# Two expert layers behind induced attention: x pooled in runs of 16 points per partition, and layer two's up weights converted by ScalarE and VectorE

## What is computed

```python
B, N, m, C = 2, 11456, 32, 128; E, F = 8, 1024

def mab(q, kv):                      # attention, scale 1/sqrt(C)
    s = scale * (q @ kv.T); a = exp(s - s.max(-1)); a /= a.sum(-1) + 1e-9
    return a @ kv
h = mab(inducing, x)                 # 32 rows per batch: the pooling over all points
x = mab(x, h).reshape(B * N, C)      # every point

# layer one: expert by cosine with expert_emb, / tau
# layer two: logits = x @ w_gate + modality_bias[modality_id]
e = argmax(logits); gate = softmax(logits)[e]
out = gate * (relu(x @ w1[e]) @ w2[e])
```

## Time and profile before

| what | us |
|---|---|
| median of 3 runs | 1101.46 (1101.04 to 1102.66) |
| the profiled execution | 1104.6 |
| its span, in which all times of the trace lie | 1102.8 |
| mean granted TensorE clock, share of full speed | 0.954 |

### The profile page before, as it was taken

The page is one execution under the profiler, slowest core; times in us unless marked ns, Lnnn a source line. Parts: engine busy times, 40 slices in busy tenths (PEclk is TensorE's granted clock), DMA queues, the critical chain, the costliest instruction groups (busy, mean ns, idle before and its releaser), DMA issues.

```text
span 1102.8 us, 27898 instructions
## 1 busy us (share of the span) xinstructions
PE 987.3 (90%) x6367; PEld 498.8 (45%) x6367; DVE 760.5 (69%) x2224; ACT 666.7 (60%) x1614; POOL 248.8 (23%) x461
## 2 busy tenths in 40 slices
PE   5566473789999999999999999999999999999887
PEld 4445231345444444444444444444454444444433
DVE  3545575657778687777777787777777777877654
ACT  3434163456666666766666666666666666667553
POOL 2759911211111111111111111111111111111100
PEclk9868786789999999999999999999999999999999
DMA  9999372101111101010111111010101111010000
GB/s 194 301 282 297 124 244 67 31 21 28 38 33 28 42 23 47 23 47 24 40 30 37 34 26 44 23 47 23 44 26 38 32 30 41 23 47 23 16 23 21
DMA packets 75163, 70.71 MB, mean 64 GB/s; under 512 B 33370, under 2 KB 61570, under 8 KB 75118
## 3 DMA queue, kind: packets, MB, share of 16 engines
q1 hardware_dynamic: 75118, 70.14, 23.8%
HBM read 40.55 MB, written 23.55 MB: 58 GB/s over the span
## 4 chain that ended last, share of the span: by engine, by line
PE 81%; DMA 8%; POOL 4%; issue 2%; DVE 2%; ACT 1%; SPq 1%; ACTq 0%; DVEq 0%; POOLq 0%
PE y L1273 43%; PE up L1296 22%; PE up L1286 7%; DMA GW<-in_x 3%; DMA wraw<-in_moe_w 2%; PE y L1350 2%; POOL wraw L472 2%; PE TB L1312 1%; DMA x_turned<-GW 1%; POOL W1B L476 1%; PE TB L1336 1%; PE SM L1324 1%; PE up L1212 1%; PE SM L1344 1%; DMA ind<-in_inducing 1%
## 5 line engine op out<-in xcount | busy, mean ns | idle before, releaser
L856 DVE SCALAR_TENSOR_TENSOR hlo<-up,hhi 128x500 f16<-128x500 f32 x736 | 494.0, 672 | 171.5 <-ACT hhi L594 168.7
L594 ACT ACTIVATE hhi<-up 128x500 f16<-128x500 f32 x736 | 424.5, 583 | 170.6 <-PE up L1296 84.6
L1296 PE MATMUL up<-ytb,W1B 128*128 (+1 forms) x1104 | 276.4, 381 | 11.9 <-issue 11.3
L1273 PE MATMUL y<-hhi,W2A 128*128 128x500 f16 x736 | 218.5, 379 | 10.4 <-DVE hlo L856 5.5
L1273 PE MATMUL y<-hhi,GW 128*128 128x500 f16 x736 | 215.4, 374 | 0.4 <-DVE hlo L856 0.4
L1296 PEld LDWEIGHTS up<-ytb,W1B 128*128 x1104 | 108.7, 99 | 149.0 <-issue 40.3
L1286 PE MATMUL up<-E4T,GW 128*128 (+1 forms) x368 | 139.4, 382 | 0.0
L1273 PE MATMUL y<-hlo,W2A 128*128 128x500 f16 x368 | 138.7, 377 | 0.0
L1273 PE MATMUL y<-hlo,GW 128*128 128x500 f16 x368 | 137.5, 374 | 0.0
L1273 PEld LDWEIGHTS y<-hhi,W2A 128*128 x736 | 68.2, 98 | 92.9 <-issue 46.2
L514 POOL TENSOR_TENSOR st<-ss,root 125x4 f32<-125x4 f32 x46 | 46.9, 1019 | 236.4 <-ACT TB L620 236.4
(11 more groups left out here) (165 smaller groups left out, 1066.0 us busy)
## 6 DMA issues: line engine op xcount, KB each, us to landing
wraw<-in_moe_w SPq DMA_DIRECT2D x24, 512.0 KB, 4.7
xth<-x_turned SPq DMA_DIRECT2D x46, 250.0 KB, 2.6
out<-yout SPq DMA_DIRECT2D x46, 250.0 KB
x_turned<-GW SPq DMA_DIRECT2D x10, 1000.0 KB, 13.4
GW<-in_x SPq DMA_DIRECT2D x10, 960.0 KB
W1B<-in_moe_w SPq DMA_DIRECT2D x8, 512.0 KB, 11.9
x_turned<-GW SPq DMA_DIRECT2D x2, 750.0 KB, 9.7
GW<-in_x SPq DMA_DIRECT2D x2, 720.0 KB
```

Source lines behind the costliest of these rows:

```text
L594: nc.scalar.activation(hhi[:, (u % UP) * CT:(u % UP + 1) * CT], ups[u % UP][:, 0:CT], ACT.Relu).then_inc(s["hi_done"], 1)
L856: nc.vector.scalar_tensor_tensor(hlo[:, o:o + CT], ups[u % UP][:, 0:CT], 0.0, hhi[:, o:o + CT], ALU.max, ALU.subtract).then_inc(s["lo_done ...
L1273: ins = mm(y[:, 0:CT], W[:, bass.ds(woff + (fb * 2 * C + o), C)], h[:, k * CT:(k + 1) * CT], start=opens and fb == 0 and n == 0, stop=fb = ...
L1296: ins = mm(ups[k][:, 0:CT], W1B[:, bass.ds(woff + (wl * F + fb * P), P)], ytb[:, bass.ds(yoff + yl * CW, CT)], start=n == 0, stop=n == 2)
```

## The change

**Points.** A quad now is one run of 2000 points (1500 in the last of a batch): partition p holds 16 consecutive points (SPANS; 12 in the last), 8 KB, and chunk k of the quad is the points 4k to 4k + 3 of each partition. Quads start at STARTS. Within a batch only quad 3 (TWICE) overlaps its successor, by 44 points; `mix_points` leaves those out by its number of rows (`rows_kept`), and `keep_twice` sums their exponentials in two reductions, once for each batch. x is loaded as one DMA on 128 partitions (three more than are used), except for the last quad, where this would pass the end of x: it keeps 120 and 5 partitions. The turned quad is stored as one row of 8 KB per partition; modalities and results follow the same order of points (`points_of`). As the starts are numbers out of a table, SP's loop over the chunks is written out.

**Weights.** `w2a` and `w2b` are loaded with 4 KB per partition (eight consecutive rows of the matrix) instead of eight rows of 512 B. The hidden columns are thereby permuted, and the up weights follow: `high_low` reads `w1b` with a stride of eight elements, and the products' halves read PSUM with the same stride.

**Conversion.** `w1b` is halved by ACT (`high_up`) and DVE (`low_up`) in the pooling loop, expert e at the end of step q = e + 3. ACT first waits for POOL to be through with `w2a` of that expert, because W1B lies over its raw weights. `w1b` of expert e is loaded at q = e + 1, beside `w2a`. POOL halves only `w2a`; its one small power for the expert norms moves behind expert 1, and the steps that make and use the norms move from q = 0, 3, 4 and 5 to q = 2, 6, 7 and 8. `inducing` is loaded first, the small constants after the first four quads.

```diff
+    SPANS = [TJ * len(gs) for gs in CHUNKS]
+    TWICE = QB - 3
+    WITHIN = [sum(TQ * n for n in SPANS[0:k]) if k <= TWICE else NT - sum(TQ * n for n in SPANS[k:QB])
+              for k in range(QB)]
+    STARTS = [b * NT + r for b in range(NB) for r in WITHIN]
+    KEPT = WITHIN[TWICE + 1] - WITHIN[TWICE]
...
+        W1B_FROM = 3
...
+        def points_of(a, g, p0, p1):
+            q, k = quad_of(g)
+            rows = a[STARTS[q] + p0 * SPANS[q]:STARTS[q] + p1 * SPANS[q]]
+            return rows.rearrange("(p t) n -> p (t n)", t=SPANS[q])[:, k * TJ * a.shape[1]:(k + 1) * TJ * a.shape[1]]
+        def pieces(q):
+            whole = TQ // 8 * 8
+            return [(0, P)] if STARTS[q] + P * SPANS[q] <= NB * NT else [(0, whole), (whole, TQ)]
+        def rows_kept(q, k, j):
+            return -(-(KEPT - k * TJ - j) // SPANS[q]) if q % QB == TWICE else TQ
...
             if kind == "w1":
-                return dst[:, bass.ds(o, F)], dst[:, bass.ds(o + F, F)], a
+                return (*(dst[:, bass.ds(o + k * F, F)].rearrange("p (f c) -> p f c", c=P) for k in range(2)),
+                        a.rearrange("p (c f) -> p f c", f=NF))
...
             def load_points(q):
-                gs, slot, whole = CHUNKS[q], q % XR_N, TQ // 8 * 8
-                for p0, p1 in ((0, whole), (whole, TQ)):
-                    r0 = row0(sp, gs[0]) + p0 * TJ
-                    points = bass.AP(xf.tensor, r0 * C, [[TJ * C, p1 - p0], [STEP * C, len(gs)], [1, TJ * C]])
-                    sp.dma_start(xr[p0:p1, slot, 0:len(gs), :], points).then_inc(s[f"x_loaded{slot}"], 16)
+                slot, n = q % XR_N, SPANS[q]
+                for p0, p1 in pieces(q):
+                    sp.dma_start(xr[p0:p1, slot, 0:n * C],
+                                 xf[STARTS[q] + p0 * n:STARTS[q] + p1 * n, :].rearrange("(p t) c -> p (t c)", t=n)).then_inc(
+                        s[f"x_loaded{slot}"], 16)
             def load_w2a(e):
-                sp.dma_start(as_w2(w2raw[:, e, :]), w2a[e, :, :].rearrange("(f p) c -> p f c", p=P)).then_inc(
+                sp.dma_start(w2raw[:, e, :], w2a[e, :, :].rearrange("(p f) c -> p (f c)", p=P)).then_inc(
                     s[f"w2a_loaded{e // 2}"], 16)
             def load_w1b(e):
                 if e >= 4:
-                    sp.wait_ge(s["w1b_steps"], 3 * (e - 3))
+                    sp.wait_ge(s["w_lo_ready"], e - 3)
...
-                sp.dma_start(XTD[gs[0]:gs[-1] + 1, :, :].rearrange("g p n -> p g n"),
-                             xT[:, q % XT_N * STREAMS:q % XT_N * STREAMS + len(gs), :]).then_inc(
-                    s[f"x_stored{q % XT_N}"], 16)
+                sp.dma_start(XTD[q, :, 0:len(gs) * 2 * CT],
+                             xT[:, q % XT_N * STREAMS:q % XT_N * STREAMS + len(gs), :].rearrange("p g n -> p (g n)")
+                             ).then_inc(s[f"x_stored{q % XT_N}"], 16)
...
                 if q + 2 < NE:
                     load_w2a(q + 2)
-                elif q + 2 < 2 * NE:
-                    load_w1b(q + 2 - NE)
-            for e in range(NQ + 2 - NE, NE):
-                load_w1b(e)
+                if 0 <= q + 2 - W1B_FROM < NE:
+                    load_w1b(q + 2 - W1B_FROM)
...
-                    sp.wait_ge(s["w1b_steps"], 3 * (e + 5))
+                    sp.wait_ge(s["w_lo_ready"], e + 5)
...
-                    sp.wait_ge(s["w1b_steps"], 3 * (e + 7))
+                    sp.wait_ge(s["w_lo_ready"], e + 7)
...
-            for e in range(NE):
-                raw = wraw[:, e % 4, :]
-                hi, lo, a = high_low(gp, "w1", W1B, e, raw)
-                gp.wait_ge(s[f"w1b_loaded{e % 4}"], 16 * (e // 4 + 1))
-                nc.gpsimd.tensor_scalar(raw, raw, S_W, None, ALU.mult).then_inc(s["w1b_steps"], 1)
...
+            def high_up(e):
+                act.wait_ge(s[f"w1b_loaded{e % 4}"], 16 * (e // 4 + 1))
+                act.wait_ge(s["w2a_steps"], 3 * (e + 1))
+                hi, _lo, a = high_low(act, "w1", W1B, e, wraw[:, e % 4, :])
+                nc.scalar.activation(hi, a, ACT.Copy, scale=S_W).then_inc(s["w_hi_ready"], 1)
...
+            def low_up(e):
+                v.wait_ge(s["w_hi_ready"], e + 1)
+                hi, lo, a = high_low(v, "w1", W1B, e, wraw[:, e % 4, :])
+                nc.vector.scalar_tensor_tensor(lo, a, S_W, hi, ALU.mult, ALU.subtract).then_inc(s["w_lo_ready"], 1)
...
-                keep_twice(q)
+                if q % QB == TWICE:
+                    keep_twice(q)
+                if 0 <= q - W1B_FROM < NE:
+                    low_up(q - W1B_FROM)
...
+                if k >= NB:
+                    hi = tmp16[:, k % 3, :].rearrange("p (f c) -> p f c", f=NF)
+                    product = gbank(k)[:, :].rearrange("p (c f) -> p f c", f=NF)
+                nc.scalar.activation(hi, product, ACT.Copy).then_inc(s["g_hi_ready"], 1)
```

More of the change, by code:

```diff
@@ L57, in attention_two_moe_kernel @@
     assert QB * STREAMS - NCB == 1 and NQ == NB * QB
+    SPANS = [TJ * len(gs) for gs in CHUNKS]
[4 more added lines that the diff above has]
+    KEPT = WITHIN[TWICE + 1] - WITHIN[TWICE]
+    assert 0 < KEPT <= TQ * SPANS[TWICE] and WITHIN[-1] + TQ * SPANS[QB - 1] == NT
     S_W = 2.0 ** 6
@@ L371, in sp_step @@
                 if xq:
-                    if not isinstance(c, int) or c > -4:
+                    if c > -4:
                         sp.wait_ge(s["chunk_scores"], c + 4)
@@ L375, in sp_step @@
                 if ry:
-                    if not isinstance(c, int) or c > -1:
+                    if c > -1:
                         sp.wait_ge(s["bias_ready"], c + 1)
                     loadm(c + 1)
-                if not isinstance(c, int) or c >= 1:
+                if c >= 1:
                     store(c - 1)
@@ L391, in _ @@
                 if e < 2:
-                    sp.wait_ge(s["w1b_steps"], 3 * (e + 7))
+                    sp.wait_ge(s["w_lo_ready"], e + 7)
                 else:
                     sp.wait_ge(s["w2b_lo_ready"], e - 1)
-                sp.dma_start(as_w2(w2s[:, e % 2, :]), w2b[e, :, :].rearrange("(f p) c -> p f c", p=P)).then_inc(
+                sp.dma_start(w2s[:, e % 2, :], w2b[e, :, :].rearrange("(p f) c -> p (f c)", p=P)).then_inc(
                     s[f"w2b_loaded{e % 2}"], 16)
             sp.sem_inc(s["out_free"], 1)
-            for c in range(-3, 1):
-                sp_step(c)
-            with sp.Fori(1, NCH - 4) as c:
-                sp_step(c)
-            for c in range(NCH - 4, NCH):
+            for c in range(-3, NCH):
                 sp_step(c)
@@ L717, in low_points @@
                                                ALU.mult, ALU.subtract).then_inc(s["lo_ready"], 1)
+            def low_up(e):
+                v.wait_ge(s["w_hi_ready"], e + 1)
+                hi, lo, a = high_low(v, "w1", W1B, e, wraw[:, e % 4, :])
+                nc.vector.scalar_tensor_tensor(lo, a, S_W, hi, ALU.mult, ALU.subtract).then_inc(s["w_lo_ready"], 1)
             def keep_twice(q):
                 v.wait_ge(s["exp_ready"], q + 1)
-                once = M * (len(CHUNKS[q]) - (q % QB == QB - 1))
-                if once < P:
-                    nc.vector.memset(twice[:, q, :], 0.0).then_inc(s["twice_clear"], 1)
-                    v.wait_ge(s["twice_clear"], q // QB + 1)
-                nc.vector.tensor_copy(twice[0:once, q, :],
-                                      pex[0:once, q % 2, CT - TQ * (CT - STEP - 1) - 1:CT:TQ]).then_inc(
+                w = pex[:, q % 2, :].rearrange("p (j q) -> p j q", q=TQ)
+                rows = [rows_kept(q, k, 0) for k in range(STREAMS)]
+                assert rows == [rows_kept(q, k, TJ - 1) for k in range(STREAMS)] and len(set(rows[1:])) == 1
+                nc.vector.tensor_reduce(twice[:, q // QB:q // QB + 1], w[:, :, rows[1]:TQ], AX.XY, ALU.add).then_inc(
                     s["twice_kept"], 1)
+                v.wait_ge(s["twice_kept"], 2 * (q // QB) + 1)
+                nc.vector.tensor_reduce(twice[0:M, q // QB:q // QB + 1], w[0:M, :, rows[0]:TQ], AX.XY,
+                                        ALU.add).then_inc(s["twice_kept"], 1)
             def maxima(q):
@@ L791, in _ @@
                                                         ALU.subtract))
+            v.wait_ge(s["exp_ready"], NQ)
             for b in range(NB):
                 link(nc.vector.memset(sums[M * len(CHUNKS[b * QB + QB - 1]):P, (b + 1) * QB - 1:(b + 1) * QB], 0.0))
-            for k in range(CT - STEP):
-                link(nc.vector.tensor_tensor(sums[:, :], sums[:, :], twice[:, :, k], ALU.subtract))
+            link(nc.vector.tensor_tensor(sums[:, TWICE:NQ:QB], sums[:, TWICE:NQ:QB], twice[:, :], ALU.subtract))
             v.wait_ge(s["pe_setup_steps"], 3)
@@ L826, in _ @@
                 v.wait_ge(s["g_hi_ready"], k + 1)
[L827 to L829 removed]
+                o, hi, product = H4[:, k % NB, :], tmp16[:, k % 3, 0:C + NE], gbank(k)[:, 0:C + NE]
+                if k >= NB:
                     e, b, q = (k - NB) // 4, (k - NB) % 4 // 2, (k - NB) % 2
```

(8 more changed lines are left out.)

90 lines of the change are left out of this document (38 added, 52 removed).

## The result

The changed kernel takes 1072.61 us (median of 4 runs, 1069.61 to 1073.95) against 1101.65 us before: a ratio of 0.9737, 95% interval 0.9712 to 0.9762. The forecast was 1069. The profiled execution took 1073.95 us, its span 1072.2.

The account below looks back on a forecast made before the run. Slow x loads at a full DMA queue were taken to bound the pooling, POOL's weight steps the products. Savings 19.3 + 3.1 + 9.7 = 32.1 us brought the median 1101.46 to 1069 us; range 1058 to 1087.

Parts of the forecast that it names:

- likeliest case: The forecast itself, all three savings together: 1063 to 1075 us, chance 0.56.
- That x moves faster: Pooling: x on 128 partitions moves at 352 GB/s instead of 203, saving 19.3 us until the last x lands.
- rival one: Pooling: x stays slow because of its source in HBM; gain 9 us, time 1092, chance 0.08.
- That the DMA sets the end of the pooling: Pooling: the load queue, 28.1 MB at 352 GB/s plus the very last x, ends it at 85 us.
- rival two: Pooling: the engines become the bound, ending it at 79 to 93 us; 1077 or 1058 to 1063, chance 0.18.
- So both fit into the wait for x: Pooling: one conversion a quad on ACT (1.05 us) and DVE (1.22, up to 2.06) is hidden, costing nothing.
- The stride "costs nothing": Products and weight conversions: reading every eighth element adds nothing on DVE or ACT, with doubling as upper bound.
- Rivals three and four: Products: the stride doubles DVE's reads, 1086 us, chance 0.10; or costs 3.5 times per element, 1111 us, chance 0.04.
- End of pooling: Last x to first product: DVE's short operations shrink with POOL idle, saving 3.1 us, bounds 0 and 4.5.
- Products: Expert products: both slots loaded beforehand, DVE sets the pace; 36.4 us instead of 46.1, saving 9.7.
- Rival five: Pooling: the change fails there, for instance ACT waits for POOL's `w2a` each quad; saves 12.8 us, 1089, chance 0.04.
- Main part: The two expert layers' chunks after the first router chain: nothing saved, 906 us.

## Why the prediction was right, and where its steps failed

**The time came out** at 1072.6 for 1069, inside the likeliest case's own range, with steps of which two were wrong and nearly cancelled: `x` and the weights moved faster than I had it, and the conversions cost what I had taken as hidden. That the first stretch still came out at 17.6 saved for 19.3 is luck.

**That x moves faster** was right, and for the reason given: rival one (x stays slow) has nothing left. The size was low, some 417 for 352 GB/s. I had taken a fast stretch of the old trace for the limit of the queue, though it was what rows of 512 B (`w2a`) and of 2000 B (the stores) made together. The Trainium skill, "HBM Reference", Specifications, gives about 425 GB/s for a core that streams alone and would have told more; the trace agrees with 423 and 431.

**That the DMA sets the end of the pooling** failed. With 420 GB/s its 28.1 MB would be over some 13 us earlier than I had it; the waits after, the share of 0.59 and the run that read `w1b` in order (last turn at 79.2 with the same loads) put the end with ACT and DVE. That is rival two's mechanism, which had 79 to 93 us; 86.7 is in its middle. Its price was not right either: it counted ACT's 1.05 us and nothing for DVE, and 6.6 to 8.0 us for a quad, where ACT's conversions of 36.1 to 94.3 us follow each other every 8.3 us. The 6.05 us for a quad, from which the lower bound of 1058 came, no row shows.

**"So both fit into the wait for x"** is the step that broke. It had two faults. The conversions' price came from the unstrided rows: 1.05 and 1.22, and it is 2.09 and 2.06. And the wait for `x` was to hide them, though the forecast itself took it away. With their price the last turn moves as the table shows (mean us of one conversion on ACT and on DVE; starts in the profiled execution):

| run | ACT + DVE | last turn | first product |
|---|---|---|---|
| `w1b` read in order | 1.07 + 1.43 | 79.2 | 98.5 |
| changed kernel | 2.10 + 2.17 | 86.7 | 111.3 |
| written with the stride | 4.78 + 5.10 | 118.8 | 153.6 |

From the first row to the second 1.77 us more for a pair, over eight pairs 14.2 us, moved the first product by 12.8; the six pairs ahead of the last turn, 10.6 us, moved that by 7.5. Most of the price shows in the time. The move into the waits gives 6.6 of the 10.7 us back.

**The stride "costs nothing".** For the products, where I had argued with a row on PSUM, this held: 36.0 us for 36.4, and 0.743 us a read. Rivals three and four had put the doubling there, and there it isn't. But I carried the same row to SBUF, of which it says nothing, and left the doubling only as a bound without ever working out what it would do to the pooling. The Trainium skill, "SBUF — State Buffer", Door 1, says that each access in a new line of 16 bytes pays, and the trace agrees for SBUF, 2.09 for 1.05 us on ACT. For PSUM it has shorter lines, of 8 bytes, and speaks of matmuls; I had stretched that to other engines, and for the reads of ACT and DVE it did not show.

**End of pooling.** Forecast 3.1 saved, 1.7 lost. The short operations did get shorter: these are the rows that answer.
```profile
L821 DVE COPY mT4b<-mT 2x128 f32<-2x128 f32 x1 | 0.2, 214 | 0.0
...
L842 DVE COPY HTr<-HT 128x256 f32<-128x256 f32 x1 | 0.3, 294 | 0.0
...
L832 DVE TENSOR_SCALAR hw<-hacc,share 128x128 f32<-128x128 f32 x2 | 0.6, 287 | 0.1
```
What I had booked as "the last weight conversion: no gain" is two pairs of strided ones, and with them the stretch takes 5.7 us more (24.6 against 18.9), some of it by the lower clock. Without them the stretch has 4.0 us less than before, the forecast's 3.1 and a little.

**Products** were right, 10.1 for 9.7, and for the reason given: the run with POOL's conversions put back has the old waits for `w1a` back.

**Rival five** did not come true. The chain names POOL's steps of `w2a` from 58.8 to 69.2 us ahead of ACT's conversion at 70.5, but ACT's own group has no idle time before it, where DVE's waits only for ACT:
```profile
L735 DVE SCALAR_TENSOR_TENSOR W1B<-wraw,W1B 128x1024 f16<-128x1024 f32 x8 | 17.3, 2167 | 9.2 <-ACT W1B L552 9.2
L552 ACT ACTIVATE W1B<-wraw 128x1024 f16<-128x1024 f32 x8 | 16.8, 2095 | 0.0
```
That conversion is expert 4's, and POOL was through with its `w2a` at 50.8 us.

**Main part.** 4.7 us saved for 0 can't be told from scatter. From the last four of PE's products with `w1a` (they begin at 169.9 us before and at 144.0 after) to the end of the span it is 932.9 us before, 928.2 after, 928.4 in the kernel before with `x` on 128 partitions, and 929.9 to 933.6 in the other ten runs: executions scatter by 5 us there, and before and after lie near its two ends. Without it the other four stretches save 25.9 us, for which the forecast had 32.1; the 6.2 between them are 1.7 in the pooling and 4.8 at its end, less 0.3 in the products and the router chain. The medians differ by 29.0; with this scatter I can't place the last 3 us.

## What to carry to other kernels

When a change takes away the bound under which other work was free, price that work again without the bound; "hidden in the wait for x" can't stand beside "x comes 19 us earlier". A row on the cost of an access holds for the memory in which it was read, so ask for a row on each memory and on reading and writing apart. And a layout that makes a DMA's rows longer should be charged to the engines that read it: here 6.8 us of gain stood against 10.7 of cost, and the order of two calls gave 6.6 back for nothing.

## What the runs showed of the hardware

- Where `x` was loaded as 120 and 5 partitions, 194 to 227 GB/s were moved, whether its rows had 2 or 8 KB. On 128 partitions, with little else in flight (5 to 7 us), it was 388 with 2 KB and 418 with 8 KB.
- Rows of 512 B for `w2a` instead of 4 KB took the mixed stream from 423 to 383 GB/s (5 to 10 us), and from 415 to 396 (20 to 70 us).
- Steps of 32 bytes in a read of f32 from SBUF made the conversion of 128x1024 1.7 to 2 times as long: ACT 1.05 to 2.09 us, DVE 1.22 to 2.06, POOL 1.04 to 2.02. From PSUM the same steps cost neither ACT (0.596 us for 128x512, 0.597 without) nor DVE (0.743, 0.744 without) anything.
- Writing f16 in steps of 256 bytes took 4.6 times as long as in order on ACT (4.78 us), and 3.9 times on DVE (4.75), which also read one input that way.
- In the changed kernel POOL's subtraction took up to 3.67 us instead of 2.13 where DVE's conversion ran beside it. In the runs that read `w1b` in order DVE's conversion took 1.43 to 1.61 us in the mean instead of 1.22. Neither moved the end here by an amount that a run separates.
